# One VectorE product per attention unit instead of three, and GpSimd adding the softmax constant for units 2 to 9

## The reference

```python
scores = scale * np.matmul(q, k.transpose(0, 1, 3, 2))
scores = np.where(mask, scores, -1000000000.0)
scores = scores - np.max(scores, axis=-1, keepdims=True)
attn = np.exp(scores)
attn = attn / (np.sum(attn, axis=-1, keepdims=True) + 1e-09)
x = np.matmul(attn, v)                       # then 1152 tokens x 512
g = softplus(x @ w_in)                       # 512 -> 2048
y = g @ w_out                                # 2048 -> 512
out = sum over 4 experts e: p[:, e] * (relu(y @ w1[e]) @ w2[e])   # 512 -> 1024 -> 512
```

## Time and profile before

| what | value |
|---|---|
| median of 3 runs | 632.71 us (632.67 to 633.68) |
| the profiled execution's own time | 633.16 us |
| its span, first to last instruction | 631.4 us |
| granted TensorE clock | 1.000 of full speed |
| TensorE matmul busy | 621.4 us, 98% |
| VectorE busy | 388.2 us, 61% |
| ScalarE busy | 276.5 us, 44% |
| GpSimd busy | 86.9 us, 14% |
| DMA | 40.78 MB |

### The profile page before, as it was taken

How to read it: one execution, slowest core, us unless ns; L and a number is a source line. 1 busy time by engine, 2 the same in 40 slices (tenths; PEclk the granted TensorE clock), 3 DMA queues, 4 the chain that set the end, 5 groups by cost and what they waited for, 6 DMA issues and landing times.

```text
span 631.4 us, 10158 instructions
## 1 busy us (share of the span) xinstructions
PE 621.4 (98%) x3892; PEld 578.6 (92%) x3892; DVE 388.2 (61%) x869; ACT 276.5 (44%) x635; POOL 86.9 (14%) x85
## 2 busy tenths in 40 slices
PE   7989999999999999999999999999999999999998
PEld 6789999999999999998998998988988988988987
DVE  5887665568645588897267267277276276376342
ACT  5887755556544465552342342332332332432410
POOL 1453333333333332000000000000000000000000
PEclk9999999999999999999999999999999999999999
DMA  8905230033200010022103003003003004000012
GB/s 326 375 36 194 75 134 1 19 115 134 67 2 0 2 33 28 7 68 94 42 0 101 34 1 100 34 1 104 31 1 113 21 1 123 12 0 1 2 51 100
DMA packets 11728, 40.78 MB, mean 65 GB/s; under 512 B 2336, under 2 KB 2592, under 8 KB 10400
## 3 DMA queue, kind: packets, MB, share of 16 engines
q1 hardware_dynamic: 11680, 40.13, 18.0%
HBM read 37.77 MB, written 2.36 MB: 64 GB/s over the span
## 4 chain that ended last, share of the span: by engine, by line
PE 95%; DMA 2%; SPq 1%; ACT 1%; DVE 0%; issue 0%
PE banks L1100 31%; PE banks L1076 28%; PE banks L1025 16%; PE banks L1045 16%; DMA part<-in_units 2%; PE banks L986 2%; PE banks L1012 1%; PE banks L999 1%; PE banks L1092 0%; SPq L315 0%; SPq L331 0%; DVE prob L681 0%; ACT prob L480 0%; SPq L323 0%; ACT sp_e L509 0%
## 5 line engine op out<-in xcount | busy, mean ns | idle before, releaser
L1100 PE MATMUL banks<-wb_hi,ehid_hi 128*128 128x512 f32 x284 | 110.5, 389 | 0.0
L1100 PE MATMUL banks<-wb_lo,ehid_hi 128*128 128x512 f32 x284 | 110.5, 389 | 0.0
L1100 PE MATMUL banks<-wb_hi,ehid_lo 128*128 128x512 f32 x284 | 110.5, 389 | 0.0
L429 POOL TENSOR_TENSOR sp_c<-sp_e,sp_c 128x384 f32<-128x384 f32 x48 | 64.1, 1336 | 135.5 <-DVE sp_c L697 135.5
L839 DVE SCALAR_TENSOR_TENSOR part<-banks,gate,part 128x512 f32<-128x512 f32 x62 | 46.6, 751 | 54.0 <-PE banks L1100 54.0
L1076 PE MATMUL banks<-T_lo,aop_hi 128*128 128x288 f32 x256 | 75.6, 295 | 0.0
L1076 PE MATMUL banks<-T_hi,aop_lo 128*128 128x288 f32 x256 | 75.6, 295 | 0.0
L1076 PE MATMUL banks<-T_hi,aop_hi 128*128 128x288 f32 x256 | 75.3, 294 | 0.0
L1025 PE MATMUL banks<-xy_hi,wa_hi 128*128 128x384 f32 x192 | 66.2, 345 | 0.0
L1045 PE MATMUL banks<-hid_hi,wb_hi 128*128 128x384 f32 x192 | 65.8, 343 | 0.0
L1045 PE MATMUL banks<-hid_hi,wb_lo 128*128 128x384 f32 x192 | 64.3, 335 | 0.0
(11 more groups left out here) (105 smaller groups left out, 1245.6 us busy)
## 6 DMA issues: line engine op xcount, KB each, us to landing
unit_in<-in_units SPq DMA_DIRECT2D x8, 1024.0 KB, 6.7
raw_a<-in_w SPq DMA_DIRECT2D x16, 512.0 KB, 3.3
raw_b<-in_w SPq DMA_DIRECT2D x16, 512.0 KB, 3.3
raw_a<-in_w_in SPq DMA_DIRECT2D x8, 512.0 KB, 5.3
raw_b<-in_w_out SPq DMA_DIRECT2D x8, 512.0 KB, 4.1
part<-in_units SPq DMA_DIRECT2D x2, 1024.0 KB, 13.4
out_dram<-part SPq DMA_DIRECT2D x8, 256.0 KB, 2.0
unit_in<-in_units SPq DMA_DIRECT2D x2, 384.0 KB, 7.2
```

The lines of the kernel that those rows point to most:

```text
L429: pool.tensor_tensor(sp_c[:, s, :], sp_e[:, s, :], sp_c[:, s, :], ALU.subtract).then_inc(lost_done, 1)
L1100: m = pe.matmul(TOKEN_BANKS[T], ehid[x][:, i, P * T:P * T + P], wb[a][:, f, :], start=(i == 0 and j == 0), stop=(i == 3 and j == 2))
```

## The change

`normalise_first(u)`, used for units 0 to 10, becomes one `tensor_tensor` over 128x384 with `rinv` broadcast along each block, in place of three `tensor_scalar` operations over 128x128. For units 2 to 9 (`EPS_AHEAD`) the constant is added to the row sums by GpSimd, which waits for `exp_done` itself and signals `eps_ahead`; VectorE waits for this and takes the reciprocal. Units 0, 1 and 10 to 23 keep VectorE's addition. On GpSimd the additions stand in the list ahead of the halves: units 2, 3 and 4 ahead of half 0, units 5, 6, 7, 8 and 9 ahead of halves 1, 2, 3, 4 and 5.

```diff
+        EPS_AHEAD = range(2, SCORED)
...
+            def add_eps(u):
+                pool.wait_ge(exp_done, u + 1)
+                pool.tensor_scalar(rowsum[:, u % 3, :], rowsum[:, u % 3, :], EPS, None, ALU.add).then_inc(eps_ahead, 1)
+
+            add_eps(2)
+            add_eps(3)
             for i in range(len(FIRST_SPLIT) - 1):
+                add_eps(4 + i)
                 pool.wait_ge(wa_hi, i + 1)
                 up_low_half(i // 2, i % 2)
             for i, unit in zip(range(len(FIRST_SPLIT) - 1, 2 * len(FIRST_SPLIT)), (7, 8, 8, 9, 9, 9)):
+                if i in (4, 5):
+                    add_eps(unit + 1)
                 pool.wait_ge(norm_done, unit + 1)
...
             def row_inverse(u):
                 dve.wait_ge(exp_done, u + 1)
-                dve.tensor_scalar(rowsum[:, u % 3, :], rowsum[:, u % 3, :], EPS, None, ALU.add).then_inc(eps_done, 1)
-                dve.wait_ge(eps_done, u + 1)
+                if u not in EPS_AHEAD:
+                    dve.tensor_scalar(rowsum[:, u % 3, :], rowsum[:, u % 3, :], EPS, None,
+                                      ALU.add).then_inc(eps_done, 1)
+                if u in EPS_AHEAD:
+                    dve.wait_ge(eps_ahead, u - EPS_AHEAD[0] + 1)
+                else:
+                    dve.wait_ge(eps_done, u + 1 if u < EPS_AHEAD[0] else u + 1 - len(EPS_AHEAD))
                 dve.reciprocal(rinv[:, u % 3, :], rowsum[:, u % 3, :]).then_inc(rinv_done, 1)
...
             def normalise_first(u):
                 dve.wait_ge(rinv_done, u + 1)
-                for w in range(3):
-                    m = dve.tensor_scalar(prob[:, u % 3, w, :], prob[:, u % 3, w, :], rinv[:, u % 3, w:w + 1], None,
-                                          ALU.mult)
-                m.then_inc(norm_done, 1)
+                p = prob[:, u % 3, :, :]
+                dve.tensor_tensor(p, p, rinv[:, u % 3, :].rearrange("p (w o) -> p w o", o=1).to_broadcast([P, 3, P]),
+                                  ALU.mult).then_inc(norm_done, 1)
```

More of the change, by code:

```diff
@@ L253, in two_stage_mlp_after_window_attention @@
         eps_done = sem("eps_done")
+        eps_ahead = sem("eps_ahead")
         rinv_done = sem("rinv_done")
```

## The result

The changed kernel takes 634.05 us (median of 20 runs, 632.71 to 635.88), the kernel before 632.96 (20 runs, 632.64 to 633.71): a ratio of 1.0017, with the 95% interval 1.0010 to 1.0024. That is 1.1 us more, slower clear of noise in these runs and still under the 0.2% that the prediction set. The time lies inside the range, 0.45 above the predicted 633.6. Its profiled execution took 634.4 with a span of 632.6, where the forecast was 634.1 and 632.3.

A forecast was written before the change was run, and what follows sets the result against it. TensorE, busy 621.4 of 631.4 us, bounds the kernel; GpSimd delays of 0.44, 0.3, 0.1 and 0.25, less 0.15 at A, give about +0.9, so the median goes from 632.71 to 633.6 us, range 632.4 to 634.4.

The forecast's parts named there:

- A: Start of VectorE's activation(0,0), said to set TensorE's time from the weighing of unit 10 on; forecast +0.9 us, to 34.8.
- W: Start of TensorE's weighing of unit 10, 3.89 us after A; forecast to move from 37.72 to 38.6 us.
- Rival 4: At unit 10's product: the single product ends the first gap and GpSimd is not late, so faster, 632.1 us; chance 0.08.
- rival 3: Before unit 10's weighing: meetings mostly missed by timing, A moves 0 to 0.4 us, 632.7 to 633.1; chance 0.15.
- H: Start of TensorE's scores of unit 10, the event from which the study, after measuring, counts times; not a forecast claim.
- Rival 5: VectorE's product with a broadcast operand runs slower than 0.55 us, say twice; joins rival 3 or 2, no own chance.
- GpSimd's start: GpSimd's five pieces before lost(0,0) start 0.44 us later, because halves 5 and 6 wait behind unit 9's addition.
- unit 9's product and the cast: These VectorE operations meet GpSimd's halves and delay GpSimd: +0.3 us for the product, +0.1 for the cast.
- unit 10's product: VectorE's single product for unit 10 meets a running GpSimd piece and delays GpSimd by 0.25 us more than before.
- A after `lost(0,0)`: VectorE's activation(0,0) follows GpSimd's lost(0,0) by 0.05 us after its end instead of 0.20, taking 0.15 off the delay.
- nothing before 20.95 us counts: Before TensorE's scores of unit 8, a load sets the time, so VectorE savings for units 0 to 5 win nothing.
- rival 2: Same place, full price per meeting or a dearer addition: A moves 1.3 to 1.8 us, 634.0 to 634.5; chance 0.27.

The follow-up runs named there:

- e3: The changed kernel, but VectorE keeps unit 9's addition too, so nothing stands ahead of half 5: 632.77 us, ratio 0.9994.
- e8: The changed kernel with GpSimd's addition for unit 9 issued behind half 6 instead of ahead of half 5: 632.77 us, ratio 0.9999.
- e2: The changed kernel with the three products per unit kept as before, so only GpSimd's additions are new: 634.05 us, ratio 1.0016.
- e10: The changed kernel plus one extra 128x256 GpSimd operation just before lost(0,0): 634.88 us, ratio 1.0030.
- e1: The kernel before with only the single product per unit; VectorE keeps all additions: 632.20 us, ratio 0.9994.
- e11: e10 plus nine matmuls of zeros on TensorE just before the weighing of unit 10: 634.33 us, ratio 1.0018.
- e5: The changed kernel with GpSimd's lost(0,0) moved ahead of halves 8 and 9: 632.68 us, ratio 1.0001.

## Why the prediction was right, and where it was not

**The place was right.** I had said that `add_eps(9)`, issued ahead of half 5, makes GpSimd bring `lost(0,0)` late, and that A and W follow. e3 and e8 take that one cause away in two ways and the loss goes; e2 has it alone and keeps it; e10 adds to it and W follows one for one. Rival 4 (faster) and rival 3 (hidden) are out for this stretch: H to W grew by 1.22 and 1.23 in two pairs of traces. Rival 5 is out by the row of the product:

```profile
L697 DVE TENSOR_TENSOR prob<-prob,rinv x11: 557/559/920, 8.4 to 31.1; 128x384 f32<-128x384 f32 x11
```

Least, median and longest of its 11 executions in ns: 0.56 us save where it meets GpSimd.

**The terms**, read in the second trace of the changed kernel against the second of the kernel before, both from H:

```profile
27.58 0.23 POOL L448 TENSOR_SCALAR rowsum<-rowsum 128x3 f32<-128x3 f32 x1 [2.17 <-ACT prob L491]
27.88 2.62 POOL L435 TENSOR_TENSOR wa_lo<-raw_a,wa_hi 128x256 fp32r<-128x256 f32 x3
30.46 1.63 POOL L442 TENSOR_TENSOR wb_lo<-raw_b,wb_hi 128x256 fp32r<-128x256 f32 x2
32.05 1.72 POOL L435 TENSOR_TENSOR wa_lo<-raw_a,wa_hi 128x256 fp32r<-128x256 f32 x2
33.73 1.01 POOL L431 TENSOR_TENSOR sp_c<-sp_e,sp_c 128x384 f32<-128x384 f32 x1
```

```profile
26.21 1.43 POOL L433 TENSOR_TENSOR wa_lo<-raw_a,wa_hi 128x256 fp32r<-128x256 f32 x2 [1.31 <-DVE prob L681]
29.00 0.84 POOL L433 TENSOR_TENSOR wa_lo<-raw_a,wa_hi 128x256 fp32r<-128x256 f32 x1 [1.35 <-DVE prob L681]
29.80 1.54 POOL L440 TENSOR_TENSOR wb_lo<-raw_b,wb_hi 128x256 fp32r<-128x256 f32 x2
31.29 1.42 POOL L433 TENSOR_TENSOR wa_lo<-raw_a,wa_hi 128x256 fp32r<-128x256 f32 x2
32.67 1.00 POOL L429 TENSOR_TENSOR sp_c<-sp_e,sp_c 128x384 f32<-128x384 f32 x1
```

| term | predicted | measured |
|---|---|---|
| GpSimd's start: half 5 at H-0.56, two halves of 1.40, so half 7 at H+0.84 instead of H+0.25 | +0.44 | +0.59 |
| unit 9's product and the cast: three halves take 2.58 from start to next start, not 1.40 + 0.80 | +0.40 | +0.38 |
| the two `wb_lo` halves: 1.59, not 1.49 | 0 | +0.10 |
| unit 10's product: the last two halves take 1.68, not 1.38 | +0.25 | +0.30 |
| `lost(0,0)` | +1.09 | +1.37 |
| A after `lost(0,0)`: 1.05, not 1.20 | -0.15 | -0.15 |
| A, and with it W | +0.94 | +1.22 |

The size that was off most is the first: I took 0.2 us for the addition with its handover, and it is 0.30 from its start to half 5's (27.58 to 27.88), for an operation of 0.23. It lies just above the upper bound of 0.29 that I had drawn from the select. The prediction's 0.2 was no more than a choice between a memset and a select, and the `wb_lo` halves were put at nothing. W fell on 38.67, a tenth from the forecast's 38.6, with an increment that was 0.28 too small: H happened to be 0.25 earlier in that execution than in the trace that I had. That match is luck in the last two or three tenths.

By the Trainium skill (SBUF, State Buffer, section Who interferes with whom), with the full 0.55 us for each product, my estimate would have been near +1.4. The measured +1.22 lies between that and the +0.9 of the rows. The full price is not borne out: unit 9's product and the cast together took 0.38 us from GpSimd and unit 10's product 0.30, not 0.55 each. Nor is the prediction's reading right that the two operations do not overlap at all: they overlap in part.

One sign of being wrong was put badly. I had written that half 5 must not start before 27.8, in absolute time. In the first trace it starts at 26.64, because the whole head is early. Taken from H it starts at H-0.56 in both traces; the forecast's 28.0 is H-0.69.

**The step that was wrong** is "nothing before 20.95 us counts". It holds where the loads land late, as they did in the one trace that I had. Where they land early, a shorter head is not lost in the wait for a load. A sign of it stood in my own rows: of the three waits for normalised scores, 1.7 us in all, only one is unit 10's; the other two, 0.25 and 0.34 us, lie before 20.95. The second trace of each kernel shows late landings: scores of unit 8 at 20.69 behind a wait of 1.31, and at 21.00 behind one of 0.78, and from there to H 7.75 us in both. The first trace of the changed kernel and e1's show early ones (19.34 and 19.27, no wait). The traces also show what the head wins ahead of this load. From the scores of unit 6 until TensorE could begin those of unit 8 (their start less the wait) it is 4.26 and 4.31 us in the kernel before (from 16.30 and 15.91) and 3.75 and 3.87 in the changed one (from 15.59 and 15.51), and the wait of 0.34 us before the transpose of unit 5 is gone. That makes 0.4 to 0.6 us, which the wait for the load swallows when the load is late. What the whole head is worth with early loads is not settled, since no trace shows the kernel before with early loads. The runs give a hint. The 20 runs of the changed kernel at a mean clock of 0.999 or 1.000 form two groups, 632.68 to 632.97 (12 of them) and 633.70 to 634.22 (8); the second trace, with late loads, belongs to the upper one (634.15), and the first, less the 1.5 us of its clock (634.4 - 1.5 = 632.9), to the lower. If the groups are early and late loads, the change costs about 1 us with late loads (634.15 against 633.16 and 633.20, all profiled) and little with early ones, where the second such time is known only from runs without a trace (those of the kernel before begin at 632.42, the changed kernel's at 632.68). That is inference from groups; no experiment separated it, and the traces account for 0.4 to 0.6 us of it.

**The step that was missing** is TensorE's clock. I had priced a pause at its length, and had even put it at 1.5 us where it is 2.1 (the transpose of unit 10 comes 0.45 us earlier after H than before, H+4.80 against H+5.25, and not 0.2, and W 0.3 later than forecast). A pause of 2.1 us was followed by a fall in the first trace and by none in the second, and a fall costs 1.50 us more (2.71 to 4.21 from W to the transpose of unit 11). With 10 of 30 runs at the lower mean clock that is about 0.5 us in the mean (10/30 x 1.5). The runs show it: those 10 lie at 634.4 to 636.51, the others at 632.68 to 634.22. This term pushed part of the runs into rival 2's 634.0 to 634.5 and beyond. Rival 2's own mechanism, meetings at full price, is not what did it.

The median of 634.05 is thus a mixture: about +1.2 at W, some of it back in the head in some runs (0.4 to 0.6 us by the traces, up to 1 by the groups), 1.5 on top in a third of them. The mechanism at W is shown; that the forecast of the median came within half a microsecond is in part luck, two omissions of opposite sign. In the ten runs beside the second trace they gave a median of 632.87, 0.7 under the forecast.

**The pauses.** Before the transpose of unit 10 I had said little or nothing: 0.32 and 0.36. Before the weighing of unit 9 there is a new one of 0.41 and 0.33 that I had not named; it costs nothing at W, where TensorE waits anyway. ScalarE waits 2.19 and 2.23 us before `hidden_high(0,0)`, as I had said (more than 2).

## What to carry to other kernels

An operation moved to an idle engine costs by its place in that engine's list: ask which work stands behind it, when its input is there, and what the engine did in that time before. The same 0.23 us addition cost 0.91 us more ahead of half 5 than behind half 6. A longer wait of TensorE can cost more than its length, because its clock may fall after it (1.5 us here, in 10 of 30 runs), and then only in a share of the runs: look at the spread and the granted clock of each run, not at the median alone. And "this part waits for a load anyway" rests on where one execution's loads landed; before a gain is written off for it, see whether the wait is there in a second trace.

## What the runs showed of the hardware

- A load of the head landed at least 1.3 us apart in two executions of one kernel (scores of unit 8 at 19.34 without a wait, and at 20.69 after 1.31 us of one).
- The same pause of 2.11 to 2.12 us before the weighing was followed by a granted clock of 0.81 over 37 to 46 us in one execution and of 1.00 in the other. A wait of 1.32 us for a load in e11 was followed by a fall too. What decides between them stays open. Over all kernels without fillers 20 of 47 runs have the lower mean clock where TensorE's longest wait from H to W is 1.68 to 2.12 us, and 11 of 155 where it is 0.45 to 1.42 us.
- The addition of 128x3 on GpSimd takes 227 ns, 0.30 us to the next start; VectorE's reciprocal of unit 9 starts 0.41 us after ScalarE's last operation for its exponentials (27.49 to 27.90), against 0.23 in the kernel before (27.76 to 27.99).
- VectorE's product with the broadcast operand takes 559 ns for 128x384, like the two-input operations of that size without it (0.55).
- In e5, where GpSimd does pieces back to back, the waiting product of VectorE ends 0.42 us after the piece in progress (33.58 against 33.16), and the next VectorE operation is held by the next piece: 1.10 and 1.08 us for two operations of 0.55.
